# V of the chunked attention loaded as full 64-row blocks over 128 partitions, one transfer per unit

## What is computed

```
for c in range(nc):                      # chunks of 32 query rows
    l_start = max(0, c_start - 16)
    r_end = min(S, c_end + 8)
    k_full = concat([mem_k, k[l_start:r_end]])      # 8 memory rows + up to 56
    v_full = concat([mem_v, v[l_start:r_end]])
    scores = scale * q_c @ k_full.T
    a = softmax(scores)
    out[c_start:c_end] = a @ v_full
```

## Time and profile before

| | us |
|---|---|
| median of 3 runs | 791.99 (790.97 to 792.47) |
| profiled execution, its time | 793.11 |
| profiled execution, its span | 791.4 |
| attention stage within it, to the last gate values | 123.0 |
| choice of the first expert's tokens, to its first matmul | 123.0 to 169.2 |
| experts and dense layer | 169.2 to 791.4 |

### The profile page before, as it was taken

The page is one execution under the profiler, slowest core; times in us unless marked ns, Lnnn a source line. Parts: engine busy times, 40 slices in busy tenths (PEclk is TensorE's granted clock), DMA queues, the critical chain, the costliest instruction groups (busy, mean ns, idle before and its releaser), DMA issues.

```text
span 791.4 us, 18169 instructions
## 1 busy us (share of the span) xinstructions
PE 707.6 (89%) x7116; PEld 615.8 (78%) x7117; DVE 566.3 (72%) x2069; ACT 356.6 (45%) x567; POOL 322.3 (41%) x241
## 2 busy tenths in 40 slices
PE   5698894179979999999989999999999999999992
PEld 3476673168969888898979897988898989898882
DVE  5598885878688778877886888687869787641150
ACT  2487784423157325713561365147414731562270
POOL 2122203685066307712751385157404730672011
PEclk9799997569999999999999999999999999999997
DMA  8799979150133013302320331033113311330001
GB/s 235 229 256 260 264 270 359 54 181 19 50 97 107 28 54 112 102 28 74 114 81 28 94 119 54 27 112 108 62 33 105 117 53 54 108 107 27 1 13 41
DMA packets 24382, 83.84 MB, mean 106 GB/s; under 512 B 4032, under 2 KB 4096, under 8 KB 24320
## 3 DMA queue, kind: packets, MB, share of 16 engines
q0 software_dynamic: 13056, 46.14, 18.4%
q1 hardware_dynamic: 11264, 36.91, 16.0%
HBM read 70.46 MB, written 12.58 MB: 105 GB/s over the span
## 4 chain that ended last, share of the span: by engine, by line
PE 63%; DVE 9%; DMA 8%; POOL 8%; issue 6%; ACT 3%; SPq 0%; POOLq 0%; DVEq 0%; ACTq 0%
PE bank L581 17%; PE bank L583 16%; PE bank L582 16%; DMA raw<-w,w_idx 6%; POOL wl L1410 6%; PE bank L506 3%; DMA vr<-v_in 2%; PE banks L487 2%; PE bank L462 2%; PE bank L472 1%; POOL raw L1404 1%; DVE z L1224 1%; PE bank L498 1%; PE banks L610 1%; PE banks L594 1%
## 5 line engine op out<-in xcount | busy, mean ns | idle before, releaser
L1410 POOL TENSOR_TENSOR wl<-raw,wh 128x1024 fp32r<-128x1024 f32 x60 | 146.5, 2442 | 21.2 <-ACT wh L796 20.4
L1404 POOL DMA_INDIRECT raw<-w,w_idx x60 | 64.9, 1081 | 158.5 <-DVE w_idx L1139 121.2
L581 PE MATMUL bank<-xh,wh 128*128 128x384 f32 x256 | 90.8, 355 | 3.5 <-POOL wl L1410 3.3
L581 PE MATMUL bank<-hh,wh 128*128 128x384 f32 x256 | 90.5, 354 | 0.0
L583 PE MATMUL bank<-xh,wl 128*128 128x384 f32 x256 | 86.9, 339 | 0.0
L582 PE MATMUL bank<-xl,wh 128*128 128x384 f32 x256 | 86.9, 339 | 0.0
L582 PE MATMUL bank<-hl,wh 128*128 128x384 f32 x256 | 86.4, 338 | 0.0
L583 PE MATMUL bank<-hh,wl 128*128 128x384 f32 x256 | 86.4, 337 | 0.0
L796 ACT ACTIVATE wh<-raw 128x1024 fp32r<-128x1024 f32 x60 | 63.4, 1056 | 44.4 <-DMA raw<-w,w_idx 44.2
L581 PE MATMUL bank<-wout_h,uh 128*128 128x512 f32 x192 | 78.7, 410 | 0.2
L581 PE MATMUL bank<-win_h,yh 128*128 128x512 f32 x192 | 77.2, 402 | 0.0
(11 more groups left out here) (216 smaller groups left out, 1702.0 us busy)
## 6 DMA issues: line engine op xcount, KB each, us to landing
unit<-qk_in SPq DMA_DIRECT2D x24, 768.0 KB, 10.1
vr<-v_in SPq DMA_DIRECT2D x48, 130.0 KB
x_rows<-x_keep SPq DMA_DIRECT2D x20, 256.0 KB, 3.7
prep_first<-w_in SPq DMA_DIRECT2D x4, 512.0 KB, 6.3
vr<-v_mem SPq DMA_DIRECT2D x32, 32.5 KB
x_rows<-x_sb SPq DMA_DIRECT2D x4, 256.0 KB, 3.8
prep_first<-w_out SPq DMA_DIRECT2D x2, 512.0 KB, 8.8
prep_rest<-w_out SPq DMA_DIRECT2D x2, 512.0 KB, 10.0
```

The source lines that it names most:

```text
L581: nc.tensor.matmul(bank, stat_h, mov_h, start=first, stop=False)
L1404: gp.indirect_dma_start(stage(s, c), None, table, bass.IndirectOffsetOnAxis(ap=w_idx[:, c % WCH:c % WCH + 1], axis=0))\
L1410: gp.tensor_tensor(wl[:, c % WCH, :], stage(s, c), wh[:, c % WCH, :].bitcast(F32), ALU.subtract)\
```

## The change

All 64 rows of every chunk and head half are prepared in memory (so 24 of 64 rows are there twice, and the memory rows are in each block), and V of a unit is one transfer over all 128 partitions with 4160 bytes each. The copies on ACT and DVE and their two semaphores go, the separate transfers of memory rows and the 25th V transfer go, and `values` of a unit waits for that unit's own V transfer. V bytes per unit become 520 KB; they were 260 KB plus 65 KB in four units of six.

```diff
-        def next_front(engine, copy, a, u):
-            ...
-            own, after = slice(64 * a, 64 * a + FRONT), slice(64 * a + CHUNK, 64 * a + CHUNK + FRONT)
-            s = CPT * (u % DEEP)
-            if s + CPT < RING:
-                last = copy(vr[after, s:s + CPT, :, :], vr[own, s + 1:s + CPT + 1, :, :])
-            else:
-                copy(vr[after, s:RING - 1, :, :], vr[own, s + 1:RING, :, :])
-                last = copy(vr[after, RING - 1, :, :], vr[own, 0, :, :])
-            last.then_inc(v_next[a], 1)
...
                 if u >= DEEP - 1:
                     sp.wait_ge(pv_ps, u - DEEP + 2)
-                slots = slice(CPT * (u % DEEP), CPT * (u % DEEP) + (CPT if u < NT else 1))
-                for a in range(2):
-                    if u % TPB < DEEP and u < NT:
-                        sp.dma_start(vr[64 * a + 64 - MEM:64 * a + 64, slots, :, :].rearrange("p c h d -> p (c h d)"),
-                                     v_mem[u // TPB, a, :, :]).then_inc(v_loaded[u % DEEP], 16)
-                    own = vr[64 * a:64 * a + CHUNK, slots, :, :].rearrange("p c h d -> p (c h d)")
-                    sp.dma_start(own, v_in[u, a, :, 0:own.shape[1]]).then_inc(v_loaded[u % DEEP], 16)
+                slots = slice(CPT * (u % DEEP), CPT * (u % DEEP) + CPT)
+                sp.dma_start(vr[:, slots, :, :].rearrange("p c h d -> p (c h d)"), v_in[u, :, :])\
+                  .then_inc(v_loaded[u % DEEP], 16)
...
-            for u in range(NT):
+            for u in range(NT - DEEP):
                 if u + DEEP + 1 < NT:
                     load_qk(u + DEEP + 1)
-                if u + DEEP <= NT:
-                    load_v(u + DEEP)
+                load_v(u + DEEP)
...
-            def values(i, r):
+            def values(i, r, n):
                 pe.wait_ge(pT_sb, i + BLANK_PT)
-                for a in range(2):
-                    pe.wait_ge(v_next[a], i + 1)
+                pe.wait_ge(v_loaded[r], 16 * n)
...
-                    next_front(act, lambda to, of: nc.scalar.activation(to, of, ACT.Copy), 1, i)
...
-            nc.vector.memset(vr[0:64, RING - CPT:RING, :, :], 0.0).then_inc(v_next[0], 1)
-            nc.vector.memset(vr[64:128, RING - CPT:RING, :, :], 0.0).then_inc(v_next[1], 1)
+            nc.vector.memset(vr[:, RING - CPT:RING, :, :], 0.0).then_inc(v_loaded[DEEP - 1], 16)
...
-                next_front(ve, lambda to, of: nc.vector.tensor_copy(to, of), 0, u)
```

More of the change, by code:

```diff
@@ L47 @@
 SCALE = 1.0 / float(D) ** 0.5
-FRONT = LEFT + RIGHT
 QW, KW, VW = HP * P, HP * CPT * WIN, CPT * HP * (D + 1)
@@ L99, in rounds_in, with build @@
     return ROUNDS_NONE if last else ROUNDS_FIRST if first else ROUNDS
-def build(nc, qk_in, v_in, v_mem, w_gate, w1, w2, w_in, w_out, g_ln, out):
+def build(nc, qk_in, v_in, w_gate, w1, w2, w_in, w_out, g_ln, out):
     ctx = ExitStack()
@@ L210, in build @@
         logits_ps = sem("logits_ps")
-        v_next = [sem(f"v_next{a}") for a in range(2)]
         dve = sem("dve")
@@ L339, in build @@
         O_BANK = [KF % 3, (KF + 1) % 3, (KF + 2 + KD + 2 * TILES) % 3]
-        def v_count(u):
-            return sum(64 if n % TPB < DEEP and n < NT else 32 for n in range(u % DEEP, u + 1, DEEP))
         def prep_high(n):
@@ L519, in step @@
                 if not known or i <= NT:
-                    values(i, (r - 1) % DEEP)
+                    values(i, (r - 1) % DEEP, n)
             pe.wait_ge(consts, 1)
@@ L527, in _ @@
             for i in range(NT, NT + 3):
-                step(i, i % DEEP, 0)
+                step(i, i % DEEP, NT // DEEP + 1)
             pe.wait_ge(gate_sb, NT + BLANK_GATE)
@@ L1501 @@
     v_p = padded(v_1, D + 1)
-    v_u = np.zeros((NT + 1, H, P, D + 1), v.dtype)
-    for u in range(NT + 1):
-        part = v_p[:, P * u:P * u + P]
-        v_u[u, :, :part.shape[1]] = part
-    v_u = v_u.reshape(NT + 1, HP, 2, CPT, CHUNK, D + 1).transpose(0, 2, 4, 3, 1, 5).reshape(NT + 1, 2, CHUNK, VW)
     m_1 = np.ones((B, H, MEM, D + 1), v.dtype)
     m_1[..., :D] = mem_v
-    m_u = m_1.reshape(B, HP, 2, MEM, D + 1).transpose(0, 2, 3, 1, 4)[:, :, :, None]
-    m_u = np.repeat(m_u, CPT, axis=3).reshape(B, 2, MEM, VW)
+    v_w = np.stack([v_p[:, CHUNK * c:CHUNK * c + WIN] for c in range(NT * CPT)]).reshape(NT, CPT, H, WIN, D + 1)
+    v_w[:, :, :, WIN - MEM:] = np.repeat(m_1, TPB, axis=0)[:, None]
+    v_u = v_w.reshape(NT, CPT, HP, 2, WIN, D + 1).transpose(0, 3, 4, 1, 2, 5).reshape(NT, P, VW)
     arrays = {
@@ L1513 @@
         "v_in": v_u,
-        "v_mem": m_u,
         "w_gate": np.asarray(inputs["moe_w_gate"]).reshape(KD, P, E).transpose(1, 0, 2),
```

## The result

The changed kernel takes 781.94 us in the median of 4 runs (780.61 to 783.15), the kernel before 792.00. The ratio is 0.9854, with a 95% interval of 0.9832 to 0.9877. So the change gains 7 to 13 us with the intervals taken together; the forecast was 6.8. In the medians it is 10.1 us the first time and 7.7 the second (791.17 and 783.47). The first ratio puts the time at 780.4, just under the range that began at 780.5.

What follows compares the result with a forecast made beforehand. It took slow V transfers to hold up the attention stage in the first 123 us, PE's own work bounding the rest. From 793.1 profiled, -3.8 (steady part) and -3.0 (start) gave 786.3; the median stands 1.1 lower, 785.2 us, range 780.5 to 790.5.

Steps and rivals of the forecast that it cites:

- Cause of the slow V: Attention-stage loads: V is slow because its transfers span 32 or 64 partitions; over 128, a unit takes 3.2 us.
- the far bound: Attention-stage loads: if V stays at 185 GB/s, a unit takes 4.81 us.
- Steady part: Attention steps 4 to 24: PE's wait for V ends, 80.07 us become 76.3; 3.8 us go, bounds 3.3 and 4.5.
- Start: First attention steps: second instruction stop shrinks (-2.6) and PE's clock recovers (-0.4); 3 us go, bounds -6.4 to +1.8.
- The stops cannot go: Attention start: PE's three instruction stops, 9.2 us, remain because the code is as long; their size hangs on the queue.
- Behind the stage: Between attention and first expert: stores, dense pieces and POOL's splitting come earlier, so nothing is added to the sum.
- This cover only grows. So the stage's gain reaches the first expert whole.: Before the first gather: POOL already stood 7.5 us waiting for token numbers, so its splitting costs nothing of the gain.
- Only the steady part gains: Rival, attention start: queue as full as before, stops stay or grow to +1.8; 788.2 to 790.0 us, chance 0.13.
- The stops vanish: Rival, attention start: stops are only a matter of the queue, 9.2 + 1.3 us go too; 777.7 us, chance 0.04.
- The gain is given back: Rival, behind the attention stage: PE's clock falls to half again; 790.5 to 793 us, chance 0.07.
- V stays slow: Rival, attention loads: V's rows or their number cause the low rate; 795 or 802 us, chance 0.08.

Runs made afterwards that it cites:

- the two splits: Changed kernel with V of a unit in two transfers: over 64 partitions each (808.56 us), or over all 128 partitions with half the columns each (782.53 us).
- e1_split64: Changed kernel, but V of a unit comes in two transfers of 64 partitions each, same bytes; 808.56 us, ratio 1.0248.
- e10_paced: Changed kernel with V of unit 3 and q, k of unit 4 held until unit 2's scores, later transfers until unit 3's; 783.22 us, ratio 0.9897.
- e12_pool_later: Changed kernel, but POOL's first subtraction waits until DVE is in the second digit of the search, about 1 us later; 782.23 us, ratio 0.9892.
- e13_changed_again: Changed kernel unmodified, timed once more beside the kernel before on the same chip; 783.47 us, ratio 0.9889.
- e4_psum_small: Changed kernel, but DVE's small operands in the choice of tokens lie in the accumulator memory, not the on-chip buffer; 780.80 us, ratio 0.9845.

## Why the prediction was right or wrong

**Cause of the slow V: right, and shown** by the two splits. The rate was 418 to 424 GB/s (forecast: 408 to 421 for q and k and the dense pieces, 378 as the low bound), 3.2 us a unit. The 185 GB/s that I took for V alone was V mixed with q and k; alone it was 229. The 218 GB/s that the prediction took from the Trainium skill (SBUF — State Buffer, Door 1: The DMA port swizzle) stands against this 229, and against 233 in e1_split64, and not against 185. With 229 the far bound would have been 4.25 us a unit and not 4.81, still above a step of PE. That e1_split64 came out at 4.85, near the bound as stated, is luck: 185 was itself the rate of a mix, and mixes are slower than their parts.

**Steady part: right in kind, 0.8 us too small.** The term "twenty steps of 3.73 with four turns of 0.43 are 76.3" measured 75.4. The step is 3.69 us: I took all of 3.73 for PE's own work and gave the copies no price beside it, though I had it as a bound (4.5 us; 4.65 measured, just beyond it). Every wait for V went.

**Start: right in size, wrong in the parts.** I put 3.0 us, measured 3.7. I left the first stop as it was and put the second at 2.6 us; the first went to 0.30, the second only to 4.34, the third to 0.61. My two reasons, a short queue for the second and nothing for the others, fit none of them; each packet of instructions simply came earlier. The stops alone gave 4.0 us, where I had 2.6; all else at the start, where I had the clock at -0.4, became 0.3 longer, and step 2's gate product still takes 1.87 us (1.83 before). That the size came out near is in part luck. "The stops cannot go" is borne out as far as it was tried: in e10_paced the second stop is 1.60 us though its packet had started at 16.12 us and no data moved.

**Behind the stage: the step that failed.** "This cover only grows. So the stage's gain reaches the first expert whole." I looked at POOL's split only as work that has to end before the gather. It is also what DVE's chain runs into: 4.5 us lost before (0.6 in `e_hot`, 2.0 in `w_idx`, 1.9 in `mask`), 2.6 after. Because the dense layer's pieces, and with them POOL's split, came 2.7 us earlier relative to the gate values, the chain got 2.0 us shorter. The sum had nothing for it. The rows were there, `w_idx` at 2.26 us for four elements, and I did not ask why. e12_pool_later shows that this term could as well have been smaller.

Together these three are the whole difference to 6.8 us in the profiled executions: 0.8 + 0.7 + 2.0 = 3.5, and 10.3 measured. The second timing's 783.47 us lies inside the range, although its profile has the same three stages, summed, to within 0.2 us: the two timings differ in what scatters behind the first gather. The bounds of the two terms alone reach down to 781.1, so the fast end of the range, 780.5, had no term behind it.

**The rivals.** "Only the steady part gains" fell: the start gained too, and the trace passed the 358 GB/s of the Trainium skill (DMA: Bandwidth & Descriptors, Specifications) with 418 over 14 us. "The stops vanish" did not happen: 5.25 us remain, and every stop ended at least 2.2 us behind its packet. "The gain is given back" by the clock: such falls occur, in the kernel before too. The one in e13_changed_again went with 2.1 us up to the second expert's gather; on the mean of the profiled runs the part behind the first gather is as long with the change as without it. "V stays slow" did not happen, but e1_split64 built its case: I had priced 795 at 4.81 us a unit and 802 at 259 GB/s, and it took 803 to 811 at 4.85. I had let the late stream act at its end alone; with a ring of four units every transfer that is late makes the next ones be sent later, since they wait for PE.

## What to carry to other kernels

Compare GB/s at a full DMA share between transfers of different shape: if one shape moves half as much, its partitions are the first suspect, and more bytes over all 128 can be cheaper than fewer over 32 or 64. When an edit moves a stage in time, look not only at who waits for it but at which long instructions of POOL it now lays beside a chain of small ones on DVE; a small instruction that takes two microseconds is the sign. And a stop of PE on first passes through new code ended, in every kernel here, 2.2 to 2.8 us behind the start of a 16 KB packet of instructions: look for that packet first. Of three schedules that held transfers back none brought the stage's end forward.

## What the runs showed of the hardware that I had not expected

- Transfers over 128 partitions passed 418 GB/s over 14 us; V as two over 64 each, with the same bytes, passed 233 alone and brought the mix with q and k to 272 GB/s.
- A small DVE instruction took 2.1 to 2.4 us in place of 0.2 when it met a 2.3 us subtraction of POOL; with the small operands in the accumulator memory (e4_psum_small) the same instructions took 0.18 to 0.35.
- PE went on 2.2 to 2.8 us after the start of a 16 KB packet of its instruction queue, at every stop of the start and with a full or an idle queue; it stood 1.60 us in e10_paced while no data moved.
- Narrow and wide transfers mixed were slower than the rates of each alone give: 4.85 us a unit in e1_split64, and not 4.2.
- One and the same kernel differed by 4.3 us in two executions whose first 149 us were equal to 0.2 us; in the slower one PE's clock was granted at 0.60 from 182 to 186 us, in the faster one at 1.00.
